# First item's rows by a ones matmul in place of the last two blocks' scatter and reload

## The reference, cut to what matters

```python
x = attention(q, k, v)                    # top-32 of 576 keys, 1152 tokens x 512
h = x @ w_in; g = maximum(h, 0) + alpha * minimum(h, 0)
x = g @ w_out                             # these rows are called x2 below
noisy = x @ w_gate + log1p(exp(x @ w_noise)) * noise     # 8 experts
top2, weights = two best experts of each token, softmax of their two scores
for e in range(8):                        # w1[e]: 512 x 1024, w2[e]: 1024 x 512
    rows = tokens with e among their two
    out[rows] += weight * (maximum(x[rows] @ w1[e], 0) @ w2[e])
```

## Time and profile before

| | us |
|---|---|
| median of 3 runs | 758.64 |
| lowest, highest | 755.74, 759.49 |
| the profiled execution | 760.67 |
| its span in the profile | 758.9 |
| PE busy in the span | 664.5 (88%) |
| DVE, ACT, POOL busy | 521.5, 465.2, 392.8 |

### The profile page before, as it was taken

The page is one execution under the profiler, slowest core; times in us unless marked ns, Lnnn a source line. Parts: engine busy times, 40 slices in busy tenths (PEclk is TensorE's granted clock), DMA queues, the critical chain, the costliest instruction groups (busy, mean ns, idle before and its releaser), DMA issues.

```text
span 758.9 us, 13760 instructions
## 1 busy us (share of the span) xinstructions
PE 664.5 (88%) x4660; PEld 564.7 (74%) x4660; DVE 521.5 (69%) x1103; ACT 465.2 (61%) x878; POOL 392.8 (52%) x435
## 2 busy tenths in 40 slices
PE   2467767999989999999999998369999999999993
PEld 2355656887867888888887777258989989989992
DVE  5799997888779989898989043454555554555520
ACT  5588866777887777777877545614554544535511
POOL 3488899678788677776787634400202202202112
PEclk9987998999999999999999999759999999999998
DMA  9759446643507536244644749380638448366222
GB/s 307 309 185 414 132 167 210 236 169 141 217 17 268 183 127 239 99 192 154 249 140 174 278 182 385 148 291 1 188 118 277 130 160 275 93 213 208 88 32 35
DMA packets 39607, 140.95 MB, mean 186 GB/s; under 512 B 10800, under 2 KB 11824, under 8 KB 35504
## 3 DMA queue, kind: packets, MB, share of 16 engines
q1 hardware_dynamic: 35168, 130.25, 47.5%
q0 software_dynamic: 4384, 9.98, 5.8%
HBM read 113.70 MB, written 45.73 MB: 210 GB/s over the span
## 4 chain that ended last, share of the span: by engine, by line
PE 70%; POOL 11%; DVE 5%; issue 4%; ACT 4%; DMA 4%; POOLq 0%; ACTq 0%; SPq 0%; DVEq 0%
PE bank L1125 12%; PE bank L974 11%; PE ps_scores L1111 9%; PE bank L935 7%; PE bank L1111 6%; PE bank L912 6%; PE bank L1130 4%; PE bank L940 3%; PE ps_scores L865 3%; POOL expo L1567 3%; PE bank L896 3%; DMA q_raw<-q_rows_dram 2%; PE bank L952 2%; DVE top L414 2%; PE bank L1093 1%
## 5 line engine op out<-in xcount | busy, mean ns | idle before, releaser
L1709 POOL DMA_INDIRECT out_dram<-ye,xe x24 | 42.8, 1783 | 219.1 <-ACT ye L1475 214.2
L414 DVE MAX8 top<-rest 128x8 f32<-128x576 f32 x216 | 152.2, 745 | 0.0
L1567 POOL TENSOR_TENSOR expo<-scores,expo 128x576 f32<-128x576 f32 x72 | 103.6, 1440 | 68.1 <-ACT scores L1195 68.0
L426 DVE MATCH_REPLACE8 rest<-top,rest 128x576 f32<-128x576 f32 x144 | 105.7, 741 | 0.0
L974 PE MATMUL bank<-w_out_high,g_parts 128*128 128x512 f32 x288 | 100.2, 410 | 0.0
L1125 PE MATMUL bank<-w_hi,he_t 128*128 128x512 f32 x256 | 91.9, 400 | 0.0
L604 DVE TENSOR_TENSOR w_lo<-raw,w_hi 128x1024 fp32r<-128x1024 f32 x64 | 77.8, 1225 | 19.5 <-ACT w_hi L1419 18.4
L912 PEld LDWEIGHTS bank<-v,prob_t 128*64 128x64 f32 (+1 forms) x1440 | 57.4, 145 | 30.2 <-ACT prob_t L1222 15.6
L912 PE MATMUL bank<-v,prob_t 128*64 128x65 f32 (+1 forms) x1440 | 73.1, 241 | 5.8 <-ACT prob_t L1222 5.8
L414 DVE MAX8 top<-scores 128x8 f32<-128x576 f32 x72 | 52.6, 746 | 33.7 <-ACT scores L1161 33.3
L935 PE MATMUL bank<-w_in_parts,x_t 128*128 128x512 f32 x272 | 71.2, 405 | 2.2 <-DMA w_in_parts<-w_parts_dram 2.2
(11 more groups left out here) (192 smaller groups left out, 1606.3 us busy)
## 6 DMA issues: line engine op xcount, KB each, us to landing
w_in_parts<-w_parts_dram SPq DMA_DIRECT2D x16, 2048.0 KB, 7.9
raw<-w_dram SPq DMA_DIRECT2D x64, 512.0 KB, 10.8
x_sorted_dram<-x_sorted_dram SPq DMA_DIRECT2D x7, 2570.0 KB, 10.9
w_parts_dram<-w_in_parts SPq DMA_DIRECT2D x4, 2048.0 KB, 10.1
q_raw<-q_rows_dram SPq DMA_DIRECT2D x18, 256.0 KB, 5.0
xe<-x_sorted_dram SPq DMA_DIRECT2D x8, 514.0 KB, 4.6
w_in_raw<-w_in_dram SPq DMA_DIRECT2D x4, 1024.0 KB, 11.0
w_out_raw<-w_out_dram SPq DMA_DIRECT2D x4, 1024.0 KB, 15.8
```

Of the source, the lines that this page charges most:

```text
L414: nc.vector.max(dst, src).then_inc(chain if r < ROUNDS - 1 else dve_top, 1)
L426: nc.vector.match_replace(rest[:, k, :], top[:, (n + k) % 4, 8 * r:8 * r + 8], src, LOWEST).then_inc(chain, 1)
L1567: nc.gpsimd.tensor_tensor(expo[:, n % 4, :], scores[:, n % SBUFS, :], expo[:, n % 4, :], ALU.mult).then_inc(pool_prob, 1)
```

## The change

The first item no longer gets the rows of blocks 7 and 8 through `x_sorted`. SP loads its 320 rows as soon as the scatters of blocks 0 to 6 have landed (`xe_first`). Slots that blocks 7 and 8 fill still hold zeros then. PE puts three things on top of each other in four PSUM banks (`first_bank`), already transposed: `early_rows`, the loaded rows times the identity, and `block_at_slots(0)` and `(1)`, the rows of block 7 and of block 8 times a matrix (`slot_hot`) that has a one where a token's slot in expert 0's region is the column's number. `slot_hot` is one DVE instruction (`hot_slots_of`) from a row of the numbers 0 to 319 (`slots_row`), which POOL counts out once with an iota (`row_count`) and DVE casts. The rows of the two blocks are split into parts (`high_x2`, `low_x2`). The scatters of blocks 7 and 8 stay; their numbers and weights are loaded later into the first item's rows.

Further moves: POOL scatters the second experts of the first `FRONT` = 4 blocks as soon as the best ones of these four have landed. The weight pieces of the first item are spread: ACT casts 0 to 3 ahead of the last copy of x2, 4 and 5 behind `softplus`, 6 behind `gap_exp`, 7 behind the rows. DVE subtracts 0 to 3 ahead of the scores of block 8 and 4 ahead of its slots, POOL subtracts 5 to 7 (`POOL_PIECES`). `count_items` (how many pairs of items) is split from `list_items` (which), and only the latter, with the slots and weights of block 8, comes behind the first item's rows on DVE.

```diff
+            def hot_slots_of(b, n):
+                nc.vector.tensor_scalar(slot_hot[n], slots_row, x_place_one[:, 0:1], picked[:, 0, b:b + 1], ALU.is_equal,
+                                        ALU.mult).then_inc(hot_slots, 1)
...
             last_prelu(3)
+            dve.wait_ge(row_count, 1)
+            step(v3.tensor_copy(slots_row, slots_int))
             score_tokens(EARLY, EARLY + 1, 1)
...
             place_block(EARLY, 1, ps_pt4)
+            for c in range(4):
+                low_weights(c, 0, c + 1)
+            low_x2(1, x2_now[:, 0:MODEL])
             score_tokens(BLOCKS - 1, BLOCKS, 2)
             pick_experts(BLOCKS - 1, BLOCKS, 2)
-            weights_of(BLOCKS - 1, BLOCKS, 2, x2[:, BLOCKS - 1:BLOCKS, WEIGHT], x2_now[:, WEIGHT:])
-            place_block(BLOCKS - 1, 2, ps_pt)
+            low_weights(4, 0, 5)
+            dve.sem_inc(dve_wl, POOL_PIECES)
+            place_last(BLOCKS - 1, 2, ps_pt)
+            count_items()
+            for n in range(3):
+                first_low_xe(n)
             list_items()
-            for c in range(8):
-                low_weights(c, 0, c + 1)
-            for t in range(3):
-                low_xe(0, t)
+            slots_block(BLOCKS - 1, 2)
+            weights_of(BLOCKS - 1, BLOCKS, 2, x2_first[1][:, WEIGHT:], x2_now[:, WEIGHT:])
...
+            sp.wait_ge(scattered_front, 16 * FRONT)
+            sp.wait_ge(scattered[0], 16 * (EARLY - FRONT))
+            sp.wait_ge(scattered[1], 16 * EARLY)
+            sp.dma_start(xe[:, 0, 0:2, 0:MODEL], ...).then_inc(xe_first, 16)
+            sp.dma_start(xe[0:WIDE, 0, 2, 0:MODEL], ...).then_inc(xe_first, 16)
...
+            def block_at_slots(n):
+                pe.wait_ge(dve_x2_low, n + 1)
+                pe.wait_ge(hot_slots, n + 1)
+                for k in range(MK):
+                    for a in range(2):
+                        mm = pe.matmul(first_bank[k][:, 0:GROUP], x2_parts[n][a][:, k * P:(k + 1) * P], slot_hot[n],
+                                       start=(n == 0 and a == 0), stop=(n == 1 and a == 1))
...
+            pe.wait_ge(route, mark["placed1"])
+            block_at_slots(0)
             x2_transpose(j, ps_t, chunks=4 * j + 4)
-            pe.wait_ge(act_h1, 4 * j + 4)
             gates(j, ps_h[:, 0:2 * EXPERTS], x2_t.rearrange("p (k n) -> p k n", k=MK))
+            early_rows()
             pe.wait_ge(act_relu, 4 * BLOCKS)
             rank(2, ps_pt)
+            block_at_slots(1)
...
-            for t in range(EARLY):
+            for t in range(FRONT):
                 scatter(1, t, x2[:, t, :])
+            pool.wait_ge(scattered[0], 16 * (EARLY - FRONT))
+            nc.gpsimd.tensor_copy(x2[:, FRONT:EARLY, WEIGHT], weight[:, FRONT:EARLY]).then_inc(weights_moved, 1)
+            for t in range(FRONT, EARLY):
+                scatter(1, t, x2[:, t, :])
+            pool.wait_ge(pe_ht1, 4 * (BLOCKS - 1) + 3)
+            nc.gpsimd.iota(slots_int, pattern=[[1, GROUP]], base=0, channel_multiplier=0).then_inc(row_count, 1)
+            def first_low_weights(c):
+                pool.wait_ge(act_wh, c + 1)
+                at = slice(c * PIECE, (c + 1) * PIECE)
+                nc.gpsimd.tensor_tensor(w_lo0[:, at], raw0[:, at], w_hi[0][:, at].bitcast(F32),
+                                        ALU.subtract).then_inc(pool_wl, 1)
+            for c in range(8 - POOL_PIECES, 8):
+                first_low_weights(c)
```

More of the change, by code:

```diff
@@ L846, in _ @@
             load_weights(e, 1)
+            sp.wait_ge(scattered[0], 16 * (BLOCKS - FRONT))
+            sp.wait_ge(scattered[1], 16 * BLOCKS)
+            sp.dma_start(xe[:, 0, 0:2, ID:], x_sorted[0:2 * P, ID:].rearrange("(t p) n -> p t n", p=P)).then_inc(xe_in[0], 16)
+            for rows in (slice(0, WIDE), slice(WIDE, 2 * WIDE)):
+                sp.dma_start(xe[rows, 0, 2, ID:], x_sorted[2 * P:GROUP, ID:]).then_inc(xe_in[0], 16)
             load_rows(r, 1)
@@ L1147, in item @@
                 second(EK - 1)
-            pe.wait_ge(route, mark["items"])
+            pe.wait_ge(route, mark["pairs"])
             more = pairs_before_last(pe)
-            for t in range(3):
-                xe_transpose(0, 0, 0, t)
             each_item(pe, more, item)
@@ L1448, in _, with first_high_xe @@
             last_high_g(j, 3)
+            act.wait_ge(pe_first, 4 * BLOCKS)
+            for c in range(4):
+                high_weights(c, 0, 0)
             copy_x2(j, last=True)
             copy_x2_t(j, x2_t, ps_t)
+            high_x2(1, x2_now[:, 0:MODEL], act_x2, j + 1)
             copy_gates(j, ps_h[:, 0:2 * EXPERTS])
             softplus(j, j + 1, 2)
+            high_weights(4, 0, 0)
+            high_weights(5, 0, 0)
             gap_exp(j, j + 1, 2)
-            act.wait_ge(pe_first, 4 * BLOCKS)
-            for c in range(8):
-                high_weights(c, 0, 0)
+            high_weights(6, 0, 0)
+            def first_high_xe(n):
+                act.wait_ge(pe_xet, n + 1)
+                if n < 2:
+                    nc.scalar.copy(xe_t[:, 0, n, :], first_bank[n][:, 0:GROUP]).then_inc(act_xet, 1)
+                else:
+                    nc.scalar.copy(xe_t[:, 0, 2:4, :], ps_scores[:, :, 0:GROUP]).then_inc(act_xet, 1)
+            for n in range(3):
+                first_high_xe(n)
+            high_weights(7, 0, 0)
             def high_xe(g, t):
@@ L1496, in item @@
                     high_weights(7, 1 - par, after)
-            act.wait_ge(route, mark["items"])
+            act.wait_ge(route, mark["pairs"])
             more = pairs_before_last(act)
-            for t in range(3):
-                high_xe(0, t)
             each_item(act, more, item)
@@ L1716, in _ @@
             pool.wait_ge(out_blank, 16)
[L1717 removed]
+            pool.wait_ge(route, mark["pairs"])
             each_item(pool, pairs_before_last(pool), item)
```

104 lines of the change are left out of this document (83 added, 21 removed).

## The result

| | before | after |
|---|---|---|
| median of the runs, us | 758.82 (20 runs) | 755.65 (20 runs) |
| lowest, highest | 755.1, 761.33 | 752.91, 758.25 |
| the profiled execution, its span | 760.67, 758.9 | 754.44, 752.5 |
| ratio of times | | 0.9965, 95% interval 0.9951 to 0.9979 |

The change takes 2.7 us off (1.6 to 3.7 by the interval). The two profiled executions differ by more, 6.4 us of span. Of these, 3.6 us are already there when `second_layer(8, 2)` ends on PE (475.06 before, 471.42 after); over all the profiled executions of this study that moment lies anywhere between 469.5 and 476.4. So I measure from that moment, called **A** from here on. The **hole** is the stretch from A to the first matmul of the first item: 28.74 us before (475.06 to 503.80) and 26.90 us after. From A to the end of the span it is 283.8 and 281.1 us, a gain of 2.7, which agrees with the times.

The account below looks back on a forecast made before the run. PE bounds the item loop, so its start sets the end: 12.1 us gained minus 6.1 lost leaves 6.0, cut to 2.5 by DVE and POOL hindering each other; 758.2 profiled, 756.1 median, own range 754 to 758, overall 751.5 to 759.0.

Parts of the forecast that it names:

- the hold: Behind block 8's experts, DVE's small operations wait for POOL's weight pieces; gain falls from 6.0 to 2.8 or 2.2, taken 2.5.
- scoring of block 7 later, from A: DVE waits for POOL's iota before scoring block 7, starting at 476.6 where it was 471.94: 4.7 us late.
- second layer starts later, from A: PE stands ahead of rank(1), so second_layer(8, 3) starts at 479.2 in place of 475.26: 3.9 us late.
- its low clock: After PE's pause the last second layer runs partly at half clock: 1.5 us more, between 0 and 2.9.
- block 7's matmuls ahead of the transposes: Block 7's eight matmuls on PE precede the transposes of block 8's x2: 0.7 us more (0.5 to 1.5).
- picked experts to first item, without a hold: From block 8's picked experts to the first item: 6.2 us where 18.3 stood, without mutual hindrance, a gain of 12.1.
- first item to the end: The item loop is bound by PE, so moving its start moves the end by as much.
- The late iota: POOL's iota stands behind all 14 early scatters, until 476.0, so DVE scores block 7 4.7 us late.
- No hindrance: Rival: POOL's pieces and DVE's small operations behind block 8's experts pass each other; gain 6.0, 752.6 us; chance 0.25.
- The iota is not late: Rival: scatters land or issue faster, PE has no pause ahead of rank(1); 4.4 us less, 751.7 us; chance 0.07.
- The second item's weights: Rival: their late loads hold PE in the first item about 8 us; 5.5 us slower, 764.1 us; chance 0.06.
- The low clock in the first item: The first item starts at PEclk 0.5 for its first 5 us or so, as before.

Follow-up runs that it names:

- e2: The changed kernel, with POOL's three weight pieces split only once DVE is done with block 8's weights; ratio to before 0.9927.
- e9: The changed kernel, with 19 unused matmuls of 512 columns on PE filling its pause ahead of rank(1); ratio to before 0.9910.
- e1: The changed kernel, with POOL's iota counted out ahead of its first scatter; ratio to before 0.9893.
- e6: The changed kernel with FRONT = 7, so all second scatters wait for all seven best ones; ratio to before 0.9986.
- e4: The kernel before, with four of eight weight casts and low pieces moved ahead and no ones matrix; ratio to before 0.9975.
- e10: e1 plus 12 unused matmuls of 512 columns on PE between the last gates and the loaded rows; ratio to before 0.9883.
- e3: The changed kernel with the iota early, POOL's pieces behind block 8's weights and the loaded rows behind rank(2); ratio to before 0.9911.
- e11: e3 plus 16 unused matmuls of 512 columns on PE ahead of rank(2); ratio to before 0.9867.
- e5: e1 plus 21 unused matmuls of 512 columns on PE between gates(8) and the loaded rows; ratio to before 0.9865.

## Why the prediction was right

The forecast was 756.1 us and a gain of 2.5 by the hold between DVE and POOL. The kernel has 755.65 and a gain of 2.7, and the traces show the mechanism. But the terms behind it were off by up to 1.5 us each, and the errors cancelled, which is luck. By its terms the change is worth 1.8 us in the hole; the last 0.9 lie behind it and aren't shown to be its own.

| term, us | forecast | measured |
|---|---|---|
| scoring of block 7 later, from A | +4.7 | +5.9 |
| second layer starts later, from A | +3.9 | +5.4 |
| its low clock | +1.5 | +1.8 |
| block 7's matmuls ahead of the transposes | +0.7 | +0.2 |
| picked experts to first item, without a hold | 6.2 | 5.4 |
| the hold | +3.5 (3.2 to 3.8) | +3.6 |
| first item to the end | 0 | -0.9 |
| gain | 2.5 | 2.7 |

**The late iota** was right in kind, and 1.2 us too small: DVE's scoring starts at A + 2.8 where it was A - 3.1. From the landing of the fourth best scatter to the iota it took 9.4 us against a forecast 10.1, but that scatter was issued 16.6 us ahead of A in the changed kernel's execution and 18.3 in the one of before. I had taken a distance between two engines' chains from one execution as fixed. 1.6 of these 1.7 us are the clock ahead of A, which had fallen in the execution of before and not in that of the change. Where it fell in the changed order too (e2), the scatter stands 18.4 us ahead of A and the iota starts at A + 0.5; with the 9.05 us behind the picked experts the change's hole would be 26.3 there (an estimate: e2's A + 17.3 and 9.05). POOL's row shows the landing and the wait:

```profile
464.02 0.25 POOL L1804 COPY x<-weight 128x4 f32<-128x4 f32 x1 [4.29 <-DMA x_sorted_dram<-x,slot_i]
...
473.39 0.43 POOL L1814 IOTA h_sb<- 128x320 int32 x1
```

The landing itself, 9.13 us in the chain, is that of the earlier trace rows, and the iota's 0.43 us was forecast at 0.4.

**The pause and the clock.** PE stood 4.75 us. The forecast 3.9 left out that the two small matmuls of `rank(1)` run at the low clock too (0.85 us to the second layer, with little of it before). The clock term was taken as half of what a wholly slow layer would cost, from the earlier trace rows, and came out at 1.8 for 1.5; e9, which fills the pause, gives it back. Two things in it don't hold. The prediction took it that a pause of 4 us costs at least what the one before 460.45 did. But that one costs the clock in nine of the 13 executions only: 2.35 us kept it at 1.00 in e1, 2.16 us lost it before. And the price doesn't grow with the pause: 4.75 us cost 1.8, while 3.29 us (e2) and 7.20 us (e6) each cost 2.4 (5.3 us from the second layer's start to the next matmul, where e1 has 2.9).

**Block 7's matmuls and the rows.** Block 7's eight were forecast at 0.7 and cost 0.2: the experts come 7.39 us behind the second layer's end, and 7.20 before. The rows were through at 488.14, ahead of the picked experts at 489.27, as taken, because PE had its clock back (24 records in 3.1 us). e1 shows that this was luck of the late iota. With the load exposed they take 5.2 us, near the 6.3 that the prediction had as their bound.

**The hold.** This is the step on which the forecast stood, and the one that e2 decides: 3.6 us. "No hindrance", which had 0.25, is refuted: L582 and L609 last until POOL's pieces end. The prediction left open whether the ones matrix, with one SBUF tensor, would be held. It was, 2.28 us for 0.45. The Trainium skill (SBUF — State Buffer, Who interferes with whom) says so: `tensor_scalar` can take the shared ports, and an operation with two SBUF inputs contends with GpSimd's reads. The trace agrees with 2.28, 2.15 and 1.81 us (L622 beside POOL's third piece, 0.30 alone in e2), and with L590 and L701, which have an operand in PSUM and take 0.16 and 0.88 us beside POOL, as they do without it. The ends fit an L582 that handles two columns in the time of one: L622's 144 columns end 0.15 us behind POOL's piece, at which rate L582's 320 would need 0.33 us and not the 0.19 measured (an estimate from these rows). `count_items` met POOL's second piece for 2.15 us and the ones matrix its first, and neither met the third, which was cast later than I had it (piece 7 comes behind `xe_t` on ACT, and POOL starts it at 497.30); the low parts at 496.40 and 497.20 weren't held.

**The other rivals.** *The iota is not late* didn't occur. e1, which brings it about, is worth 8.1 us, 5.4 beyond the change where this rival gave 4.4, because the hold went with it. What the rival had as "about 1 us" for the rows not loaded yet was 6 us of delay to `rank(2)`. *The second item's weights* do not bound PE. SP's first load went out 5.7 us after the first item's start, near the 5 us estimated, and ACT got them in time:

```profile
508.73 1.05 ACT L1516 CAST w_hi<-raw 128x1024 fp32r<-128x1024 f32 x1 [2.96 <-DMA raw<-w_dram]
```

That cast waits 2.96 us for its load, but PE is busy in all of 501.5 to 540.

**The low clock in the first item** was forecast "as now", 5 us or so. It was 3.2, and with it the errors cancel. But its length varies from one execution to the next without the change (5.8 us before, 3.1 in e4), so this is luck and no effect that was foreseen.

## What to carry to other kernels

Where two paths of nearly equal length lead to the same point, a cut in one shows nothing until the other is cut as well: read both lengths before either is priced, and try both edits together. When a wait is added to an engine that works in order, ask what else stands on the issuing engine's queue ahead of the signal; here one iota of 0.43 us behind fourteen scatters brought the last block's experts 7 us late, and with it ahead of them the gain was three times as large. Before work is given to GpSimd, look whether VectorE issues an operation with two SBUF operands or a `tensor_scalar` on the critical path at that time, however few columns it has: here such operations cost 3.6 us. And measure a stage from more than one execution before two kernels are compared in it: the clock ahead of A moved what stands behind it by 1.6 us.

## What the hardware showed that was not expected

- An eight-column operation of 0.17 us took 2.15 us because it read two SBUF tensors beside a POOL piece, while a 128x320 operation with one operand in PSUM took its usual time 4 us later. Eight columns and 320 were held alike, until the end of POOL's piece.
- A pause on PE costs more than the pause: 4.75 us of standing added 1.8 us to the next second layer (e9), and in e1 a wait of 4.82 us added 2.2 us to the loaded rows (e10). Idle matmuls in the gap gave that back, up to 2.5 us from e3 to e11 in the hole. They need not end before the awaited event: in e9 they outlasted it by 1.0 us and still gained 2.4. In e5 they took 6.5 us and outlasted the load by 4.7, more than the clock gives back.
- Nearly the same wait of PE had two outcomes: of 13 waits of 2.06 to 2.42 us at one place in the program, nine were followed by a mean granted clock of 0.72 over 6 us and four by 1.00. The length doesn't decide it (2.35 us kept the clock, 2.16 lost it); what does stays open.
- The matmuls that were to keep the clock up can themselves start at the low one: 21 of them took 6.5 us in e5, at a granted 0.75, where 16 took 3.9 us in e11 at 1.00. In e5 PE had just stood 1.9 us for DVE, which had waited 3.4 us. What DVE waited for stays open.
